# The MLP's first product in three float32r passes, a ring of three small units, and an activation without tanh

## The reference

```python
# attention, for each batch and head
S = a_n[t] * S + k[t] v[t]^T ; y[t] = q[t] . Re(S)      # a_n complex, |a_n| <= 0.999
# MLP
h = x @ w_in                          # 3072 x 384 @ 384 x 2048
sp = np.where(h > 20.0, h, np.log1p(np.exp(np.minimum(h, 20.0))))
g = h * np.tanh(sp)
x = g @ w_out                         # 3072 x 2048 @ 2048 x 384
# experts
e_idx = argmax(x @ w_gate + modality_bias[modality_id])
out[e_idx == e] = gate * (relu(x @ w1[e]) @ w2[e])
```

## Time and profile before

| | us |
|---|---|
| median of 3 runs | 1166.32 (1156.36 to 1172.15) |
| profiled execution, its time | 1157.54 |
| its span | 1155.8 |
| TensorE busy | 1018.1 (88%) |
| ScalarE busy | 677.4 (59%) |
| VectorE busy | 559.5 (48%) |
| granted TensorE clock, mean share of full | 0.965 |

### The profile page before, as it was taken

One profiled execution on the slowest core, in us unless ns is written; L12 is line 12 of the kernel. 1 busy time (PEld: TensorE's weight loads), 2 busy tenths in 40 slices (PEclk: granted clock), 3 DMA queues, 4 the chain that ended last, 5 costly groups with the idle time before them and its releaser, 6 DMA issues.

```text
span 1155.8 us, 17734 instructions
## 1 busy us (share of the span) xinstructions
PE 1018.1 (88%) x6132; PEld 879.0 (76%) x6133; DVE 559.5 (48%) x1004; ACT 677.4 (59%) x1149; POOL 80.2 (7%) x137
## 2 busy tenths in 40 slices
PE   2469999999999999999999999998049999879996
PEld 0457777778877877878877878867049999879996
DVE  4354556555555646556555554233633333463332
ACT  4365767866877877768778666463113444444443
POOL 1000000000000000000000000000002222232222
PEclk9989999999999999999999999998569999999999
DMA  6722111121121121121121100000052111331110
GB/s 104 231 49 49 21 36 35 35 56 35 35 55 36 35 55 32 26 47 35 36 55 35 22 9 19 1 21 1 22 190 77 37 38 41 137 135 34 41 40 29
DMA packets 145356, 58.56 MB, mean 51 GB/s; under 512 B 131225, under 2 KB 140455, under 8 KB 145296
## 3 DMA queue, kind: packets, MB, share of 16 engines
q1 hardware_dynamic: 138480, 42.63, 16.2%
q0 software_dynamic: 3616, 10.43, 2.8%
q10 hardware_dynamic: 3200, 4.72, 1.1%
HBM read 48.21 MB, written 10.03 MB: 50 GB/s over the span
## 4 chain that ended last, share of the span: by engine, by line
PE 77%; ACT 9%; issue 6%; DVE 3%; SPq 2%; DMA 2%; ACTq 0%; POOL 0%; POOLq 0%; DVEq 0%
PE bank L1253 20%; PE bank L1272 15%; PE bank L1419 13%; PE bank L1430 10%; PE bank L1226 4%; PE bank L1202 3%; PE bank L1228 3%; PE bank L1194 2%; PE bank L1212 2%; ACT act_t L599 1%; SPq L389 1%; PE bank L1180 1%; PE bank L1174 1%; ACT qk_t L555 1%; ACT L532 1%
## 5 line engine op out<-in xcount | busy, mean ns | idle before, releaser
L1253 PE MATMUL bank<-x_t,w_in_sb 128*128 128x384 f32 x768 | 272.3, 491 | 0.6 <-ACT x_t L568 0.6
L1253 PEld LDWEIGHTS bank<-x_t,w_in_sb 128*128 128x128 f32 x768 | 139.0, 191 | 71.1 <-issue 1.2
L1419 PE MATMUL bank<-xg_t,w_sb 128*128 128x128 f32 x1296 | 157.5, 284 | 18.0 <-ACT he L748 16.7
L1419 PEld LDWEIGHTS bank<-xg_t,w_sb 128*128 128x128 f32 x1296 | 155.9, 200 | 19.3 <-ACT he L748 17.6
L1272 PE MATMUL bank<-w_out_hi,g_hi 128*128 128x392 f32 x384 | 149.2, 389 | 13.8 <-ACT logits L613 9.3
L593 ACT ACTIVATE hid<-bank 128x384 f32<-128x384 f32 x128 | 62.4, 488 | 138.5 <-PE bank L1253 138.1
L1272 PE MATMUL bank<-w_out_hi,g_lo 128*128 128x392 f32 x384 | 131.7, 343 | 0.0
L1272 PE MATMUL bank<-w_out_lo,g_hi 128*128 128x392 f32 x384 | 131.7, 343 | 0.0
L866 DVE TENSOR_TENSOR hid<-hid,act_t 128x1536 f32<-128x1536 f32 x32 | 56.1, 1752 | 87.4 <-ACT act_t L606 87.4
L748 ACT ACTIVATE he<-bank 128x128 f32<-128x128 f32 x216 | 59.3, 277 | 66.0 <-PE bank L1419 59.7
L1272 PEld LDWEIGHTS bank<-w_out_hi,g_hi 128*128 128x128 f32 x384 | 73.3, 191 | 20.2 <-issue 15.6
(11 more groups left out here) (199 smaller groups left out, 1760.2 us busy)
## 6 DMA issues: line engine op xcount, KB each, us to landing
w_sb<-in_moe_w_dram SPq DMA_DIRECT2D x8, 1536.0 KB, 7.1
ab<-in_a_re_dram SPq DMA_DIRECT2D x24, 192.0 KB, 3.1
ab<-in_a_im_dram SPq DMA_DIRECT2D x24, 192.0 KB, 3.4
qk_raw<-in_q_dram SPq DMA_DIRECT2D x24, 192.0 KB, 3.6
qk_raw<-in_k_dram SPq DMA_DIRECT2D x24, 192.0 KB, 3.8
v_in<-in_v_dram SPq DMA_DIRECT2D x24, 192.0 KB, 3.0
x_rows<-x_sb ACTq DMA_DIRECT2D x8, 576.0 KB, 3.4
w_out_sb<-in_moe_w_out_dram SPq DMA_DIRECT2D x2, 1536.0 KB, 9.5
```

The source lines that it names most:

```text
L1253: last = mm(bank_h[f % 2][:, 0:TT], w_in_sb[:, kk, f * P:(f + 1) * P], x_t[:, m % 2, kk], start=(kk == 0), stop=(kk == KD - 1))
L1419: last = mm(bank_h[f % 2][:, 0:P], w1_sb[par][:, kk, f * P:(f + 1) * P], xg_t[:, kk], start=(kk == 0), stop=(kk == KD - 1))
```

## The change

- `hidden` makes its product in three passes of float32r (`w_in_hi` with `x_hi`, `w_in_hi` with `x_lo`, `w_in_lo` with `x_hi`) instead of one of float32. So `w_in` is split on load (`split_w_in`, four parts of four blocks, a copy on ScalarE and a difference on VectorE), and the turned result of attention is split too: `take_yt` writes `x_hi`, and a new VectorE step at p 9, `take_low`, writes `x_lo`.
- A unit is two blocks, and three units' buffers take turns (`RING`); `act_t` has two. `second` comes six blocks late (`LAG`).
- The activation has no tanh: with e = exp(min(h, 20)) it is h * e(e + 2) / (e(e + 2) + 2). `weigh` on VectorE clamps and makes the numerator, `inverse_of` on ScalarE makes the reciprocal as exp(-ln), and `times` multiplies. So the table of tanh isn't loaded. The steps of a unit are due at new gaps, some in the next slot (`due`).
- To make room, `qk_raw`, `v_in` and `qk_hat` have one buffer instead of two, and `fresh`, `small`, `carry_row`, `y_sb` share those of others, with waits for their last use.
- SyncE issues `w_in` in four parts ahead of the first `carry_on`, and `qk_load(1)` behind it.
- The gate columns are made in gaps 1 to 9 of slot 0. The flags are counted at gaps 4, 8 and 12 of the last slot.

```diff
-    QF = 4
+    QF = 2
+    RING = 3
+    LAG = 6
+    WF = 4
...
-    STARTS = (0, 10, 21)
-    EXP_GAPS = (0, 8, 16, 23)
-    TANH_GAPS = (3, 10, 18, 25)
...
-    CLAMP_GAPS = (2, 9, 17, 24)
-    TIMES_GAPS = (6, 12, 20, 27)
...
+    STARTS = (0, 10, 20)
+    EXP_GAPS = (3, 7, 11, 17, 18, 23, 27, 31)
+    WEIGH_GAPS = (4, 8, 12, 17, 19, 24, 28, 31)
+    INV_GAPS = (7, 9, 13, 19, 21, 27, 29, 34)
+    TIMES_GAPS = (9, 10, 14, 20, 22, 28, 30, 36)
...
                 for kk in range(KD):
-                    last = mm(bank_h[f % 2][:, 0:TT], w_in_sb[:, kk, f * P:(f + 1) * P], x_t[:, m % 2, kk],
-                              start=(kk == 0), stop=(kk == KD - 1))
+                    for i, (w, x) in enumerate(((w_in_hi, x_hi), (w_in_hi, x_lo), (w_in_lo, x_hi))):
+                        last = mm(bank_h[f % 2][:, 0:TT], w[:, kk, f * P:(f + 1) * P], x[:, m % 2, kk],
+                                  start=(kk == 0 and i == 0), stop=(kk == KD - 1 and i == 2))
                 last.then_inc(h_ready, 1)
...
+            def inverse_of(u):
+                act.wait_ge(weighted, u + 1)
+                act.activation(act_t[:, u % 2], act_t[:, u % 2], ACT.Ln, scale=1.0 / CENTRE, bias=ratio_bias[:, 0:1]
+                               ).then_inc(ln_ready, 1)
+                act.wait_ge(ln_ready, u + 1)
+                act.activation(act_t[:, u % 2], act_t[:, u % 2], ACT.Exp, scale=-1.0).then_inc(inv_ready, 1)
...
-                    if g == 16 and m:
+                    if g == 2 * LAG and m:
                         take_x2(m - 1)
...
+            def weigh(u):
+                a, h = act_t[:, u % 2], hid[:, u % RING]
+                dve.wait_ge(exp_ready, u + 1)
+                dve.tensor_scalar(a, a, EXP20, None, ALU.min).then_inc(clamped, 1)
+                dve.wait_ge(clamped, u + 1)
+                dve.scalar_tensor_tensor(out=a, in0=a, scalar=2.0, in1=a, op0=ALU.add, op1=ALU.mult).then_inc(ratio_top, 1)
+                dve.wait_ge(ratio_top, u + 1)
+                dve.scalar_tensor_tensor(out=h, in0=h, scalar=1.0 / CENTRE, in1=a, op0=ALU.mult, op1=ALU.mult).then_inc(weighted, 1)
...
+            def take_low(ch):
+                m, cc = divmod(ch, CT)
+                ts = slice(cc * C, (cc + 1) * C)
+                dve.wait_ge(x_hi_ready, ch + 1)
+                dve.tensor_tensor(x_lo[:, m % 2, :, ts], bank_a[:, 0:KD * C].rearrange("p (k t) -> p k t", k=KD),
+                                  x_hi[:, m % 2, :, ts].bitcast(F32), ALU.subtract).then_inc(x_lo_ready, 1)
...
-            qk_load(1)
             decays_load(2)
-            v_load(1)
+            for n in range(NW):
+                w_in_load(n)
             carry_on(0)
             last_row(0)
+            qk_load(1)
```

More of the change, by code:

```diff
@@ L287, in handed, with due @@
             return n - n // NC
+        def due(gaps, m, g):
+            units = [(g + GAPS * late, m - late, gaps.index(g + GAPS * late)) for late in (1, 0) if g + GAPS * late in gaps]
+            return [mm * NQ + i for _, mm, i in units if mm >= 0]
         def place(gap):
@@ L384, in _ @@
             w_out_load(WL, WL)
-            for half in range(2):
-                w_in_load(half)
             sp.dma_start(mod_raw[:], modality_id.bitcast(I32).rearrange("(g p x) -> p g x", p=P, x=2)
@@ L629, in slot @@
             def slot(m):
-                before = m * NQ - 1
                 for g in range(GAPS):
@@ L645, in slot @@
                         log_mag(x + 1)
-                    if g in EXP_GAPS and before + EXP_GAPS.index(g) >= 0:
-                        exp_of(before + EXP_GAPS.index(g))
-                    if g in TANH_GAPS and before + TANH_GAPS.index(g) >= 0:
-                        tanh_of(before + TANH_GAPS.index(g))
+                    for u in due(INV_GAPS, m, g):
+                        inverse_of(u)
+                    for u in due(EXP_GAPS, m, g):
+                        exp_of(u)
                     if g in TRIG_GAPS and x < NCH:
@@ L721, in _ @@
                 slot(m)
-            last = NT * NQ - 1
-            exp_of(last)
-            tanh_of(last)
+            inverse_of(NT * NQ - 1)
             act.wait_ge(slow_known, 1)
@@ L890, in attend @@
                     state_in(ch)
+                elif p == 9:
+                    take_low(ch)
             def slot(m):
-                before = m * NQ - 1
                 for g in range(GAPS):
@@ L903, in slot @@
                         attend(ch, p)
-                    if g in CLAMP_GAPS and before + CLAMP_GAPS.index(g) >= 0:
-                        clamp(before + CLAMP_GAPS.index(g))
                     if x + 1 < NCH and p == 3:
@@ L1013, in _ @@
                 hats(x)
+                if ch == CT - 1:
+                    split_w_in(0)
             for m in range(NT):
                 slot(m)
-            last = NT * NQ - 1
-            clamp(last)
-            times(last)
-            count_flags()
+            times(NT * NQ - 1)
             dve.wait_ge(slow_known, 1)
@@ L1372, in _ @@
                 slot(m)
-            for n in range(NT * FT - 2 * QF, NT * FT):
+            for n in range(NT * FT - LAG, NT * FT):
                 second(n)
-            pe.wait_ge(flags_ready, 1)
-            mm(bank_y[:, 0:2], ones[:], flag_n[:], start=True, stop=True).then_inc(flags_counted, 1)
             pe.wait_ge(slow_known, 1)
```

294 lines of the change are left out of this document (167 added, 127 removed).

## The result

The changed kernel takes 1180.47 us (median of four runs, 1179.59 to 1181.11), the kernel before 1169.24 (four runs, 1156.36 to 1172.65): ratio 1.016, 95% interval 1.010 to 1.023. So it is slower, by 1 to 2.3%. The same kernel run again later gave 1178.98 against 1166.50, ratio 1.014 (1.007 to 1.021). The forecast was 1159, its range 1127 to 1180: missed by 21 us, half a microsecond above the range, and on the other side of no change.

A forecast was written before the change was run, and what follows sets the result against it. TensorE's own work was taken to bound the slots. Terms 7.2 + 2 + 0 - 0.6 - 7.1 - 8.8 = -7.3 us, against the median of 1166.3, gave 1159 us, range 1127 to 1180.

The forecast's parts named there:

- The product: Hidden block on TensorE: nine float32r passes, 1.57 to 1.60 us, saving 0.35 a block, 5.6 us per full slot.
- VectorE's and ScalarE's new work: Full slot: VectorE's queue holds about 71 us of 82 to 90, not the bound; ScalarE gets emptier.
- The rival with VectorE as the bound: Full slots: dependent unit operations take 1.1 us instead of 0.95, about +5 us a slot, 1191; chance 0.08.
- Walking through a full slot: Full slot: new waits sum to 8.5 us where 3.0 is idle now, giving 89.95 us, nothing gained.
- the wait at gap 12: Full slot: TensorE waits 3.3 us for the previous result's copy, queued behind other ScalarE work.
- an end of the range: Tail: the new wait of 3.0 us might also bring half clock, +2.6 us; whether it would was left open.
- Slot 0: First slot: two second blocks +3.3, 5.6 saved, new waits of about 4; +2 us (-2 to +7).
- Prologue: Before slot 0: earlier loads -2.9, take_low ahead of hats +5.0, later start of slot 0 +5.1; sum +7.2 us.
- slot 6: Slot whose last chunk has no fractions and less on ScalarE: 86.1 us, -0.6.
- last slot and tail: Last slot -7.1 us from shorter cycles and a shorter copy wait; tail 14.4 against 23.2, -8.8.
- queues keep up: Rival, all slots: TensorE stays the bound, full slots 84.5 us, 35 us less, 1124; chance 0.24.
- The chance of 0.09: Whole kernel: the forecast's probability of being slower by over 2%.

The follow-up runs named there:

- the best version: Changed kernel with x2 copies first, four unit gaps moved, w_in splits in the prologue, idle products in prologue and slot 0: 1123.04 us, ratio 0.970.
- the run with the four moved steps: Changed kernel with only four gaps of the activation's weigh, inverse and times steps moved later: 1159.43 us, ratio 0.996.
- all four edits: Changed kernel with x2 copies first, four unit gaps moved, w_in splits and the gate's first eight turns in the prologue: 1134.20 us, ratio 0.979.

## Why the prediction was wrong, by its own steps

- **The product** (1.57 to 1.60 us a block): right in the main. Passes start 0.17 to 0.18 us apart at the full clock (541.15 to 541.32 above; the median is 0.177), nine of them 1.59; in the last slot a hidden and a second block together take 3.19 instead of 3.54. The rule of the Trainium skill, page "TensorE: Matmul & The Clock Gate", section "Wait — 56ns, not 53.3ns?", would have had 0.1625 (an estimate); the trace disagrees, as the earlier trace rows did.
- **VectorE's and ScalarE's new work**: right (about 71 us of a slot predicted, 70.2 measured, 351.13 over five). The rival with VectorE as the bound did not happen; the number was slower, its reason another.
- **Walking through a full slot**: the waits are right one by one, 7.6 us in sum for 8.5. At the full clock and with the copies as late as ever, slots 1 to 5 take 448.30, and the forecast was 449.75. **The step that failed is what the wait at gap 12 costs**: I charged 3.3 us, and it costs 3.05 and the clock behind it, 10.8 us in five slots. I had the mechanism in hand, from the earlier trace rows, and wrote it down for the tail, as 2.6 us at an end of the range, where a wait is met once. The same size of wait stood in every full slot, and I didn't apply it there.
- **Slot 0, "+2 (-2 to +7)": the larger failure, 18 us.** It was summed as two seconds, the saving, and "about 4" of waits taken without a walk. The waits inside it came to 12.7 us (6.0 and 1.0 at the gate, 5.7 at the borders) where 5.5 had been, so 7 new ones for 4; the larger rest is the clock, at its lower level for 41 us, which the term put at nothing. The runs give its parts: 10 us are clock at the start and at the gate (118.2 to 108.4 with idle products), 6.4 the splits of `w_in`, by waits and the clock behind them. With both edits slot 0 took 102.6, 15.6 less, so they nearly add up. The remaining 2.4 over the 100.2 of the forecast stay open.
- **Prologue** (+7.2) +6.7, near by some luck: VectorE went on at 44.04 instead of 49.01, -5.0 for -2.9, the next chunks cost +5.2 for +5.0, and the start of slot 0 +6.4 for +5.1; **slot 6** (-0.6) +1.0, with the same clock behind a wait of 1.98; **last slot and tail** (-15.9) -13.2: a wait of 2.68 in the tail and 3.4 us at half clock, the case I left as an end (-6.2 instead of -8.8). The Trainium skill, same page, section "HAM oscillation — how this bites in real kernels", says that idle time throttles the engine; the trace agrees here (2.68 and 3.05 us of waiting, the clock at 0.5 behind both), though the page has it for longer gaps than these. Charged in slot 0 and in the full slots as well, with the prices measured since, 10 and 10.8, the forecast for the profiled execution would have been 1171 for 1179.6 measured.
- **The rivals**: "queues keep up" got 0.24. As a statement on this kernel it was false, and it is what the best version does. None of them had the clock. The chance of 0.09 was for slower by over 2%, which 1.6% is not; the upper end at 1180 was too low for a change whose whole sum rested on waits of a known size.

## What to carry to other kernels

A wait that a change adds has two prices, its own length and the lower clock behind it; before a gain on TensorE is summed, every new wait of 2 to 3 us, as they were here, has to be charged with both, and by the number of slots in which it stands. When an engine's work gets cheaper and nothing speeds up, look for a copy or a step queued behind unrelated work of the same gap: here two moves of order, with no instruction less, were worth 21 us each. Slots that differ from the usual one (here the first, with the gate and the splits) need a walk of their own, as close as that through a full slot.

## What the runs showed of the hardware

- The clock falls after waits that I had taken for too short to matter, and it depends on what lies near them. A wait of 1.98 us in slot 6 of the changed kernel, with one of 1.06 some 3 us before it, was followed by 3.4 us at 1.2 GHz; in the run with the four moved steps the same wait of 1.98 stood alone, and the clock stayed. Waits of 1.35 to 1.63 (all four edits) left it as well. Single waits of 2.70 (slot 0 of the kernel before) and of 2.68 (the tail) brought it down. In slots 1 to 5 the wait of 3.05 came behind one of 1.05. In slot 0 it fell 1.7 us behind a wait of only 1.18, among the gate's products of eight columns; in the run with the splits in the prologue, and in the one with the prologue kept busy, the same wait left it, and it fell in the next one, of 2.87.
- Twelve products whose result nobody reads keep the clock as well as real ones do, and cost next to nothing where they stand in a wait (those of the prologue had slot 0 begin at 102.2 instead of 100.5). Where the wait is shorter than they are they do cost: the last slot, with a wait of 1.12, took 1.3 us longer.
- At the lower level TensorE looks busier: in the gate's stretch of slot 0 it was busy for 10.83 of 13.70 us while it did 48 products. Its busy share hid the loss; the column of the clock showed it.
- The start of slot 0 scatters between executions of the same prologue: 100.5, 100.7, 99.7, 105.3 and 105.6 us. Both late ones had longer stretches at the lower clock in the prologue than the others (20.5 and 37.5 us in a row, against 13.7); what set these off stays open.
